# The rows of v at the sinks, loaded and split once for all eight pairs of heads

## What is computed

```python
scores = scale * np.matmul(q, k.transpose(0, 1, 3, 2))
keep = is_sink | in_window            # is_sink: pos < n_sink, n_sink = 4
scores = np.where(keep, scores, -1000000000.0)
a = np.exp(scores - np.max(scores, axis=-1, keepdims=True))
a = a / (np.sum(a, axis=-1, keepdims=True) + 1e-09)
return np.matmul(a, v)
```

## Time and profile before

| | value |
|---|---|
| median of three runs | 1254.23 us (1253.05 to 1255.44) |
| the profiled execution | 1253.09 us, span 1251.3 us from first to last instruction |
| attention | 0 to 110 us of the span |
| granted TensorE clock | 1.00 throughout, the upper level of 2.4 GHz |
| TensorE busy | 1236.2 us, 99% |
| VectorE, ScalarE, GpSimd busy | 691.7, 365.1, 535.7 us |

### The profile page before, as it was taken

The page is one execution under the profiler, slowest core; times in us unless marked ns, Lnnn a source line. Parts: engine busy times, 40 slices in busy tenths (PEclk is TensorE's granted clock), DMA queues, the critical chain, the costliest instruction groups (busy, mean ns, idle before and its releaser), DMA issues.

```text
span 1251.3 us, 18785 instructions
## 1 busy us (share of the span) xinstructions
PE 1236.2 (99%) x6446; PEld 1097.3 (88%) x6446; DVE 691.7 (55%) x1348; ACT 365.1 (29%) x832; POOL 535.7 (43%) x625
## 2 busy tenths in 40 slices
PE   7999999999999999999999999999999999999998
PEld 4558899989988999999999999999999999999997
DVE  7895734356665555555555555555555555555554
ACT  7884634312233222222222222222222222222221
POOL 7772315644444444444444444444444444444440
PEclk9999999999999999999999999999999999999999
DMA  6440000111110111111111111111111111111102
GB/s 204 156 149 18 1 1 1 34 35 34 34 35 28 38 36 36 34 34 34 34 34 34 34 34 34 34 34 34 34 34 34 34 34 34 34 34 34 35 18 101
DMA packets 57264, 53.13 MB, mean 42 GB/s; under 512 B 4352, under 2 KB 44544, under 8 KB 57216
## 3 DMA queue, kind: packets, MB, share of 16 engines
q1 hardware_dynamic: 56928, 52.19, 13.1%
q10 hardware_dynamic: 288, 0.33, 0.1%
HBM read 49.35 MB, written 3.15 MB: 42 GB/s over the span
## 4 chain that ended last, share of the span: by engine, by line
PE 95%; ACT 2%; DVE 2%; DMA 1%; issue 1%; SPq 0%; DVEq 0%; ACTq 0%
PE ps L797 30%; PE ps L798 30%; PE ps L799 30%; PE ps L722 2%; PE ps L766 1%; PE ps L742 1%; PE ps L847 1%; ACT probs L1042 1%; ACT acc L1218 1%; DVE probs L1270 1%; DMA k_sb<-kT 0%; PE ps L977 0%; DVE xw L1303 0%; ACT xw L1066 0%; DMA q_sb<-qT 0%
## 5 line engine op out<-in xcount | busy, mean ns | idle before, releaser
L1528 DVE SCALAR_TENSOR_TENSOR acc<-ps,gate_now,acc 128x512 f32<-128x512 f32 x336 | 252.1, 750 | 166.2 <-PE ps L799 162.0
L797 PE MATMUL ps<-ring 128*128 128x512 f32 x768 | 300.6, 391 | 0.0
L798 PE MATMUL ps<-ring 128*128 128x512 f32 x768 | 299.8, 390 | 0.0
L799 PE MATMUL ps<-ring 128*128 128x512 f32 x768 | 299.2, 390 | 0.0
L1200 ACT ACTIVATE sums<-ps 128x384 f32<-128x384 f32 x192 | 94.4, 492 | 597.8 <-PE ps L799 597.8
L1504 DVE TENSOR_TENSOR sums<-ps,sums 128x384 f32<-128x384 f32 x192 | 106.9, 557 | 158.2 <-ACT sums L1200 106.9
L799 PEld LDWEIGHTS ps<-ring 128*128 128x128 f32 x768 | 144.3, 188 | 30.9
L797 PEld LDWEIGHTS ps<-ring 128*128 128x128 f32 x768 | 144.2, 188 | 27.9 <-DVE acc L1524 0.4
L798 PEld LDWEIGHTS ps<-ring 128*128 128x128 f32 x768 | 144.2, 188 | 25.8
L642 POOL TENSOR_TENSOR w_raw<-w_raw 128x256 f32<-128x256 f32 x32 | 23.7, 741 | 321.3 <-PE ps L799 321.3
L797 PE MATMUL ps<-xw,ring 128*128 128x384 f32 x448 | 152.5, 340 | 0.3 <-ACT sums L1200 0.2
(11 more groups left out here) (148 smaller groups left out, 1765.2 us busy)
## 6 DMA issues: line engine op xcount, KB each, us to landing
w_in<-w_exp SPq DMA_DIRECT2D x64, 256.0 KB, 3.2
w_raw<-w_exp SPq DMA_DIRECT2D x64, 128.0 KB, 2.8
w_raw<-w_exp SPq DMA_DIRECT2D x32, 256.0 KB, 3.2
v_sb<-v SPq DMA_DIRECT2D x16, 192.0 KB
out<-acc SPq DMA_DIRECT2D x12, 256.0 KB, 2.0
q_sb<-qT SPq DMA_DIRECT2D x7, 384.0 KB, 4.4
k_sb<-kT SPq DMA_DIRECT2D x7, 384.0 KB, 4.9
k_sb<-kT SPq DMA_DIRECT2D x9, 256.0 KB, 5.7
```

The lines of the kernel that those rows point to most:

```text
L797: pe.matmul(o, ws[0], xs[0], start=first, stop=False, skip_group_check=True)
L798: pe.matmul(o, ws[0], xs[1], start=False, stop=False, skip_group_check=True)
L799: return pe.matmul(o, ws[1], xs[0], start=False, stop=last, skip_group_check=True)
L1528: dve.scalar_tensor_tensor(out=acc[:, T, :], in0=y_bank(u, T), scalar=gate_now[:, T:T + 1], in1=acc[:, T, :], op0=ALU.mult, op1=ALU.add).t ...
```

## The change

The tiles `v_sink` and `v_sink_r` get a place for each of the eight pairs (72 x 1024 elements in place of 72 x 256). Six transfers, each with four rows of all eight pairs of one head, fill them at the start; they count on a semaphore of their own. They stand on the SP queue behind the loads of v of pair 0 and of segment 0, and behind a wait for the memset of `v_sink`. That memset (now 72 x 1024) moves on GpSimd from before the masks to behind them. In pair 0 GpSimd waits for the six transfers and then runs `split_v_sinks`: it rounds all 72 x 1024 elements in one operation, and takes the rests of rows 64 to 71, 8 x 1024 elements, in a second, with a wait for its own first and one for its second. The function stands between `lay_sinks(1)` and `round_segments(0)`. `load_v` is left with one transfer, `round_v_sinks` and VectorE's `rest_v_sinks` are gone, and the wait of SP before the first load of v is gone.

```diff
-        v_sink = sb("v_sink", [SINK_ROWS, 2, P], F32, in_a)
-        v_sink_r = sb("v_sink_r", [SINK_ROWS, 2, P], F32R, in_a)
+        v_sink = sb("v_sink", [SINK_ROWS, PAIRS, P], F32, in_a)
+        v_sink_r = sb("v_sink_r", [SINK_ROWS, PAIRS, P], F32R, in_a)
...
             def load_v(p, h):
                 sp.dma_start(v_sb[:, p % 2, h, :], v[p, h]).then_inc(v_loaded[p % 2], 16)
+
+            def load_v_sinks(h):
                 for row in (0, 32, 64):
                     row += h * NS
-                    sp.dma_start(v_sink[row:row + NS, p % 2, h * DH:(h + 1) * DH],
-                                 v[p, h, 0:NS, 0:DH]).then_inc(v_loaded[p % 2], 16)
+                    sp.dma_start(v_sink[row:row + NS, :, h * DH:(h + 1) * DH],
+                                 v[:, h, 0:NS, 0:DH].rearrange("p n d -> n p d")).then_inc(v_sinks_loaded, 16)
...
-            sp.wait_ge(consts, 2)
             for h in range(2):
                 load_v(0, h)
             load_segments(0)
+            sp.wait_ge(v_sinks_clear, 1)
+            for h in range(2):
+                load_v_sinks(h)
...
-            pool.memset(v_sink[:, :], 0.0).then_inc(consts, 1)
...
+            pool.memset(v_sink[:, :, :], 0.0).then_inc(v_sinks_clear, 1)
             pool.memset(sink_cols[:, :, :].bitcast(F32), 0.0).then_inc(sinks_hi, 1)
...
-            def round_v_sinks(p):
-                pool.wait_ge(v_loaded[p % 2], 128 * (p // 2 + 1))
-                if p >= 2:
-                    pool.wait_ge(x_full, p - 1)
-                if p == 0:
-                    pool.wait_ge(consts, 2)
-                pool.tensor_scalar(v_sink_r[:, p % 2, :], v_sink[:, p % 2, :], 1.0, 0.0,
+            def split_v_sinks():
+                pool.wait_ge(v_sinks_loaded, 96)
+                pool.tensor_scalar(v_sink_r[:, :, :], v_sink[:, :, :], 1.0, 0.0,
                                    ALU.mult, ALU.add).then_inc(v_sinks_hi, 1)
+                pool.wait_ge(v_sinks_hi, 1)
+                low = v_sink_r[64:SINK_ROWS, :, :]
+                pool.tensor_tensor(low, v_sink[64:SINK_ROWS, :, :], low.bitcast(F32),
+                                   ALU.subtract).then_inc(v_sinks_split, 1)
+                pool.wait_ge(v_sinks_split, 1)
...
                 if p == 0:
+                    split_v_sinks()
                     round_segments(0)
                     rest_w_in(0)
...
                 split_sinks(p)
-                round_v_sinks(p)
...
-            def rest_v_sinks(p):
-                dve.wait_ge(v_sinks_hi, p + 1)
-                low = v_sink_r[64:SINK_ROWS, p % 2, :]
-                dve.tensor_tensor(low, v_sink[64:SINK_ROWS, p % 2, :], low.bitcast(F32),
-                                  ALU.subtract).then_inc(v_sinks_split, 1)
...
-                if t == 3 and p > 0:
-                    rest_v_sinks(p - 1)
```

More of the change, by code:

```diff
@@ L219, in solu_moe @@
         sinks_hi, sinks_split = sem("sinks_hi"), sem("sinks_split")
+        v_sinks_clear, v_sinks_loaded = sem("v_sinks_clear"), sem("v_sinks_loaded")
         v_sinks_hi, v_sinks_split = sem("v_sinks_hi"), sem("v_sinks_split")
@@ L503, in _ @@
             pool.memset(mask1[:, 0:NS], 0.0).then_inc(masks, 1)
+            pool.memset(v_sink[:, :, :], 0.0).then_inc(v_sinks_clear, 1)
             pool.memset(sink_cols[:, :, :].bitcast(F32), 0.0).then_inc(sinks_hi, 1)
-            pool.wait_ge(consts, 2)
+            pool.wait_ge(consts, 1)
             pool.affine_select(out=ident[:, :], in_=ident[:, :], compare_op=ALU.not_equal, fill=1.0,
@@ L519, in normalise @@
                 last.then_inc(probs_ready[1], 1)
-            def round_v_sinks(p):
-                pool.wait_ge(v_loaded[p % 2], 128 * (p // 2 + 1))
-                if p >= 2:
-                    pool.wait_ge(x_full, p - 1)
-                if p == 0:
-                    pool.wait_ge(consts, 2)
-                pool.tensor_scalar(v_sink_r[:, p % 2, :], v_sink[:, p % 2, :], 1.0, 0.0,
-                                   ALU.mult, ALU.add).then_inc(v_sinks_hi, 1)
+            def split_v_sinks():
+                pool.wait_ge(v_sinks_loaded, 96)
+                pool.tensor_scalar(v_sink_r[:, :, :], v_sink[:, :, :], 1.0, 0.0,
+                                   ALU.mult, ALU.add).then_inc(v_sinks_hi, 1)
+                pool.wait_ge(v_sinks_hi, 1)
[3 more added lines that the diff above has]
+                pool.wait_ge(v_sinks_split, 1)
             def split_sinks(p):
@@ L758, in pv @@
                 if b == 0:
-                    pe.wait_ge(v_loaded[p % 2], 128 * (p // 2 + 1))
+                    pe.wait_ge(v_loaded[p % 2], 32 * (p // 2 + 1))
                     if p > 0:
@@ L771, in pv_sinks @@
                 pe.wait_ge(*copied(p, SINK_USE))
-                pe.wait_ge(v_sinks_split, p + 1)
-                pe.matmul(x_psum(2, QT), v_sink_r[:, p % 2, :], sinkT[:, :],
+                pe.wait_ge(v_sinks_split, 1)
+                pe.matmul(x_psum(2, QT), v_sink_r[:, p, :], sinkT[:, :],
                           start=False, stop=True, skip_group_check=True).then_inc(x_full, 1)
@@ L788, in back @@
                     if p == 0:
-                        pe.wait_ge(consts, 3)
+                        pe.wait_ge(consts, 2)
                     turn(p, 0)
@@ L1091, in _ @@
                     act.wait_ge(small_loaded, 32)
-                    act.wait_ge(consts, 5)
+                    act.wait_ge(consts, 4)
                     act.activation(wg[:, :, WG_AT:WG_AT + EXPERTS], wg_raw[:, :, :], ACT.Copy).then_inc(wg_ready, 1)
@@ L1403, in _ @@
             copy_pT(PAIRS - 1, 2, 1)
-            rest_v_sinks(PAIRS - 1)
             solu(1)
```

## The result

The changed kernel took 1255.43 us as the median of 20 runs, against 1252.68 us for 20 runs of the kernel before. The ratio is 1.0019, with a 95% interval of 1.0012 to 1.0025: slower by some 2.4 us (1.5 to 3.1), which on this kernel is small but real. Its profiled execution took 1254.14 us with a span of 1252.4, against 1253.09 and 1251.3 before: 1.1 us more, so this one execution shows less of the loss than the medians do, which lie 2.75 us apart.

The account below looks back on a forecast made before the run. GpSimd's pair 0 work, through SP's queue and pair 2's k load, was taken to set when TensorE's full last stretch begins. +3.56 - 2.52 = +1.0 us on 1253.09 gave 1254.1, or 1255.3 for a median; range 1252.0 to 1258.0.

Parts of the forecast that it names:

- within 0.2%: Verdict on the whole time: no change larger than about 2.5 us either way, chance 0.68.
- The path: GpSimd's pair 0 to SP's wait to pair 2's k load: inserted work delays `scores(2, 0)` by its full 3.56 us.
- The 8 x 1024 operation: GpSimd's rests in pair 0: 2.36 us, drawn from two-input rows at 256 and 512 elements; bounds 1.06 and 2.56.
- The gain in the pairs: VectorE's rests gone from the pairs: five operations give back about 2.5 us in all, bounds 1.5 and 3.4.
- the distance to what is late next: Middle pairs: each removed VectorE operation returns this distance, not its duration; 0.37 us in three pairs, 0.73 and 0.67 in two.
- The wait for the six transfers: GpSimd in pair 0: transfers land by 11.4 us, GpSimd comes at 11.81, so cost nothing; bound 1.2 us.
- the landing of g_col: SP's queue in the prologue: g_col, issued behind the old six, lands at 11.4 us, so the new six should by then.
- Rival (b): Six transfers of 256-byte rows land after GpSimd comes, which waits: sum +2.3 to +3.3 us, chance 0.18.
- The moved memset: GpSimd's prologue: 0.9 us more before its first scaling, where it idles 2.28 us, and SP likely not waiting; cost nothing.
- VectorE's long hold at 13 us: VectorE may be held by GpSimd's 2.36 us operation, 1.1 us more than before; cost nothing while GpSimd is later.
- The clock: TensorE's granted clock: read as 1.00 in both stretches, with no idle time that could change it; no term given.

Follow-up runs that it names:

- x9: Changed kernel with GpSimd's 8 x 1024 two-input operation run a second time, result unused; ratio to before 1.0037, median 1257.40 us.
- x6: Changed kernel with an unused 8 x 128 operation, shaped and placed like the old rests, given back to VectorE in each pair; ratio 1.0032, median 1257.64 us.
- x2: Changed kernel with the memset of v_sink back ahead of the masks; ratio to before 1.0015, median 1255.45 us.
- x8: Changed kernel with 12 and 10 small unused transposes on TensorE ahead of two of its waits; ratio to before 1.0020, median 1254.94 us.
- x3: Changed kernel with GpSimd's two operations moved to the end of pair 0, behind split_sinks; ratio to before 1.0006, median 1253.74 us.
- x4: Changed kernel with the memset first and GpSimd's two operations at the end of pair 0; ratio to before 1.0000, median 1252.74 us.
- x1: The changed kernel run again without an edit; ratio to before 1.0019, median 1255.34 us.
- x10: Changed kernel with the memset first and GpSimd's two operations behind the rounding of segment 0; ratio to before 1.0012, median 1254.18 us.
- x5: Changed kernel with the memset first and the six transfers ahead of the loads of v and segment 0; ratio to before 1.0011, median 1254.24 us.
- x7: Changed kernel with six transfers last in the prologue, memset first, GpSimd rounding and taking rests pair by pair in idle time; ratio 0.9981, median 1250.77 us.

## Why the prediction was right, and where a term was off

The time lies in the range, the verdict "within 0.2%" fits a ratio of 1.0019 just barely, and the likeliest time, 1255.3, is near the median of 1255.43. The last is partly luck: the prediction started from a median of three runs, 1254.23, and twenty gave 1252.68. The difference is what was forecast, and there it said +1.0 us where +2.4 (1.5 to 3.1) came. The missing 1.4 us belong for the most part to things that it put at nothing: the late start of GpSimd's two operations (by the moved memset or by the landing of the six transfers, whichever comes last) and the clock.

- **The path** through GpSimd's pair 0, SP's wait and the load of k: right. In x9 2.35 us and a wait more come out as 2.37 at SP's next load, and as 2.0 to 2.3 in the time. The 8 x 1024 operation took 2.36 us, as drawn from the rows of other lengths: eight partitions are no cheaper than 128. From the one to the next operation it is 3.57 where 3.56 was said.
- **The gain in the pairs**: 2.52 said, 2.38 in the trace, 11.06 us for a pair where "about 11.0" was said. x6 takes 1.6 of it back. The reading by the distance to what is late next (TensorE's turning) gave the 0.3 to 0.4 of a pair where the operation's own duration would have given 0.5 and more.
- **The wait for the six transfers** is the term that was mis-sized: "0.4 us of cover, cost nothing", with a bound of 1.2. GpSimd, waiting for them, could start at 13.16 in x2, 13.82 in x6 and 14.60 in x8, and not at 11.4. The step that failed is the inference from the landing of g_col: one 4 KB transfer behind the old ones, of 1 KB each, said nothing on six transfers of 32 rows of 256 bytes each. Against the 11.9 at which GpSimd was to be ready that is 1.2 to 2.7 us; in three of the five traces with the changed kernel's start it is not seen as a wait, since GpSimd came late itself. Rival (b) with its sum of +2.3 comes nearest to the medians.
- **The moved memset**: "Nothing" was wrong. The step weighed it against GpSimd's idle time and SP's wait, and not against VectorE's copies, which contend with it: 1.0 us (x3 less x4). In the changed kernel it costs nothing on top that can be told, since it falls into the wait for the transfers; removing it alone gave nothing (x2).
- **VectorE's long hold at 13 us** came as 1.57 us, and stayed without cost, as said. Where the same operation stands elsewhere (x4), TensorE idles for 1.40 us behind it.
- **The clock** had no term: the prediction read 1.00 in both stretches and no idle time "of the kind that could change it". The change made such idle time. The mean granted clock is known for every execution, also for those without a trace:

| kernel | executions at 1.000 | their median | median of the others (0.995 to 0.999) |
|---|---|---|---|
| before, beside x1 to x10 | 64 of 75 | 1252.53 | 1254.77 |
| changed | 9 of 20 | 1254.50 | 1255.66 |
| changed again (x1) | 4 of 10 | 1254.56 | 1256.67 |
| x2 | 3 of 11 | 1254.28 | 1255.58 |
| x3 | 7 of 11 | 1253.73 | 1254.23 |
| x4 | 6 of 11 | 1252.68 | 1252.75 |
| x5 | 1 of 11 | 1254.24 | 1254.26 |
| x6 | 1 of 6 | 1256.17 | 1257.70 |
| x7 | 10 of 11 | 1250.57 | 1252.84 |
| x8 | 10 of 11 | 1254.93 | 1259.84 |
| x9 | 0 of 5 | | 1257.40 |
| x10 | 0 of 11 | | 1254.18 |

In the changed kernel the two groups lie 1.2 us apart, and its median lies 0.9 above that of the executions at 1.000. That is what the fall is worth here, as far as a comparison of groups can say it; in x4 and x5 they hardly differ. It also takes a part of the 1.7 us of x3 against the changed kernel: among executions at 1.000 it is 0.8. The memset's price (x3 less x4) is 1.05 among them, as before.

Counted in the one trace, whose clock was at 1.00: +1.18 ahead of the operations, +3.61 for them up to SP's next issue, -1.05 on SP's queue and in the load, -2.38 in the pairs, -0.26 behind. Sum 1.1 us, the difference of the two spans. The measured +2.4 is another 1.3 us higher than that. Some 0.9 of it is the fall of the clock in eleven of the twenty executions. Landings later than in this trace, as x6 and x8 show them, could give the rest, but no run shows when the transfers landed in the executions without a profile. That part stays open.

## What to carry to other kernels

Gathering small operations of all rounds into one at the start moves them to where nothing is pipelined yet: price the whole length on the path of the first round, and look for idle time in the rounds first. A long operation also holds whoever contends with it for its full length (2.23 us for a scaling of 0.29); with the memset first, the same work as one piece at the end of pair 0 gave 1.0000, and in eight pieces laid in idle time 0.9981. And when an edit that removes a visible stall gives nothing, look for the wait that had been behind it. Where the granted clock of every execution is known, sort the times by it before calling a rest unexplained.

## What the runs showed of the hardware

TensorE's granted clock fell to its lower level of 1.2 GHz in six of the traces (x2, x3, x5, x6, x9, x10), each time after TensorE had stood idle, for 1.3 to 4.6 us, around a late scaling or the wait for k. In x2, by stretch (the third figure from the end is the clock):

```profile
16.00:20.00 4.00, 0.98 (x7) 0.42 (x4) 1.25 (x5) 2.29 (x8) 3.91 (x5) 0.99 0.01 2
20.00:22.00 2.00, 0.40 (x2) 0.40 (x3) 0.00 (x0) 0.00 (x0) 1.81 (x5) 0.50 0.19 71
22.00:24.00 2.00, 2.00 (x9) 1.01 (x8) 1.25 (x4) 0.17 (x1) 1.29 (x4) 0.50 0.98 318
```

In the traces of before and after it was at 1.00 throughout, with TensorE idle for 1.5 us at most at a time. The length of one idle time doesn't tell the cases apart, though: it fell in x3 after one of 1.42 us and not in x8 after one of 3.30, where the transposes stood ahead of it. Where it fell at the start of pair 2 (x5, x10), for 3 to 4 us, the stretch from `scores(2, 0)` to the last pair took 61.2 us in place of 59.65.

In five traces (x1, x5, x6, x9, x10) matmuls between 11 and 18 us also took up to twice their time, while the record of the clock says 1.00: 1.97 us for eight turnings in x1, for which the changed kernel's own trace has 1.10. In that trace it is seen for the six turnings at 11.29 alone, 1.54 us in place of the 0.88 of before. No run here explains that.

A GpSimd operation on few partitions was no cheaper: 1.04 us for 72 x 1024 with one input, where 128 x 1024 took 1.056, and 2.36 for 8 x 1024 with two, which is what 128 partitions would give by the rows at 256 and 512 elements.
